# Entering the last stage of a three-stage kernel in another order: first tiles turned into two banks, two mixing tiles moved, VectorE's list rewritten

## What is computed

```python
x   = attention(q, k, v)              # 2 batches, 8 heads, window of 96 keys and 8 global keys
out = 0
for e in range(4):                    # the experts
    h = maximum(x @ w1[e], 0)         # 512 -> 1024
    out += p[:, e:e+1] * (h @ w2[e])  # 1024 -> 512
x  = out
h  = x @ w_in                         # the last stage: 512 -> 1024
sm = exp(h - max(h)) / (sum(exp(h - max(h))) + 1e-9)
s  = h * sm                           # softmax times its own argument ("solu")
ln = (s - mean(s)) / sqrt(var(s) + 1e-6) * g_ln
result = ln @ w_out                   # 1024 -> 512
```

## Time and profile before

| what | value |
|---|---|
| median of three runs | 760.61 us |
| the profiled execution, own time | 760.59 us |
| its span, first to last instruction | 758.8 us |
| TensorE busy | 745.1 us (98% of the span) |
| VectorE busy | 525.1 us (69%) |
| ScalarE busy | 220.9 us (29%) |
| GpSimd busy | 343.9 us (45%) |
| mean granted TensorE clock | 1.000 |
| last stage (first `up` to last instruction) | 605 to 758.8 us |

### The profile page before, as it was taken

How to read it: one execution, slowest core, us unless ns; L and a number is a source line. 1 busy time by engine, 2 the same in 40 slices (tenths; PEclk the granted TensorE clock), 3 DMA queues, 4 the chain that set the end, 5 groups by cost and what they waited for, 6 DMA issues and landing times.

```text
span 758.8 us, 12666 instructions
## 1 busy us (share of the span) xinstructions
PE 745.1 (98%) x3994; PEld 653.1 (86%) x3994; DVE 525.1 (69%) x1038; ACT 220.9 (29%) x418; POOL 343.9 (45%) x330
## 2 busy tenths in 40 slices
PE   9999999999999999999999999999999987999997
PEld 8888899889889988998898998989989865888885
DVE  5677767676666766666666666676677778867772
ACT  4677641111111111112111111111115643433331
POOL 4367546154451544516445164352645973442300
DMA  8746300101101001010010100100023000000001
GB/s 249 205 141 166 104 31 1 55 29 29 56 0 55 28 28 55 0 55 28 28 55 5 50 28 28 55 0 0 0 111 111 0 1 15 15 28 29 29 14 43
DMA packets 39103, 37.12 MB, mean 49 GB/s; under 512 B 14496, under 2 KB 31904, under 8 KB 39072
## 3 DMA queue, kind: packets, MB, share of 16 engines
q1 hardware_dynamic: 37472, 34.64, 14.8%
q10 hardware_dynamic: 1600, 2.10, 0.8%
HBM read 33.59 MB, written 3.15 MB: 48 GB/s over the span
## 4 chain that ended last, share of the span: by engine, by line
PE 94%; DVE 4%; issue 1%; ACT 0%; POOL 0%; POOLq 0%; DVEq 0%
PE y_ps L783 35%; PE p_ps L766 31%; PE o_ps L824 5%; PE s_ps L797 3%; PE pT_ps L807 3%; PE out_ps L1019 2%; PE out_ps L1021 2%; PE out_ps L1020 2%; PE up_ps L994 2%; PE up_ps L995 2%; PE up_ps L996 2%; PE lnT_ps L1006 1%; DVE ex L1721 1%; PE o_ps L901 1%; PE xt_ps L835 1%
## 5 line engine op out<-in xcount | busy, mean ns | idle before, releaser
L783 PE MATMUL y_ps<-w2s,hs 128*128 128x512 f32 x1152 | 289.3, 395 | 0.4 <-issue 0.3
L766 PE MATMUL p_ps<-xs,ws 128*128 128x384 f32 x1344 | 254.9, 336 | 0.0
L783 PEld LDWEIGHTS y_ps<-w2s,hs 128*128 128x128 f32 x1152 | 214.6, 188 | 41.7 <-issue 0.8
L766 PEld LDWEIGHTS p_ps<-xs,ws 128*128 128x128 f32 x1344 | 237.6, 188 | 11.0
L1430 DVE SCALAR_TENSOR_TENSOR acc<-y_ps,pr,acc 128x512 f32<-128x512 f32 x180 | 134.3, 748 | 80.1 <-PE y_ps L783 79.3
L1081 ACT ACTIVATE hs<-hs_sum 128x384 fp32r<-128x384 f32 x128 | 67.3, 526 | 354.1 <-DVE hs_sum L1398 238.9
L1417 DVE SCALAR_TENSOR_TENSOR hs<-hs_sum,hs 128x384 fp32r<-128x384 f32 x128 | 95.0, 752 | 3.8 <-ACT hs L1081 1.8
L546 POOL TENSOR_TENSOR ws_sum<-raw_sum 128x256 f32<-128x256 f32 x16 | 11.8, 738 | 147.8 <-PE p_ps L766 146.0
L577 POOL CAST w2s<-raw_sum 128x1024 fp32r<-128x1024 f32 x16 | 16.9, 1055 | 86.3 <-PE y_ps L783 86.3
L1094 ACT ACTIVATE neg_s<-neg_s,row 128x256 f32<-128x256 f32 (+1 forms) x96 | 42.1, 482 | 26.5 <-DVE row L1449 26.4
L1449 DVE CUSTOM_DVE_ANT_0 neg_s<-s_ps,bias 128x256 f32<-128x256 f32 (+1 forms) x96 | 34.3, 399 | 20.8 <-PE s_ps L797 18.6
(11 more groups left out here) (140 smaller groups left out, 967.0 us busy)
## 6 DMA issues: line engine op xcount, KB each, us to landing
raw_sum<-in_w SPq DMA_DIRECT2D x28, 512.0 KB, 3.5
qk<-in_qkW SPq DMA_DIRECT2D x24, 256.0 KB, 3.7
qk<-in_qkW SPq DMA_DIRECT2D x24, 128.0 KB, 4.1
v_sb<-in_v SPq DMA_DIRECT2D x16, 192.0 KB, 3.1
out<-o_sb SPq DMA_DIRECT2D x12, 256.0 KB, 2.0
raw_sum<-in_w ACTq DMA_DIRECT2D x4, 512.0 KB, 7.9
raw_sum<-in_w_in SPq DMA_DIRECT2D x1, 2048.0 KB, 7.6
wout_lo_a_sum<-in_w_out SPq DMA_DIRECT2D x1, 1792.0 KB, 7.7
```

The costliest lines, as they stand in the source:

```text
L766: mm = nc.tensor.matmul(bank, ws[slot][:, w, part, kk, :], xs[:, 2 * bt + kk, x, part, :], start=(kk == 0 and w == 1 and x == 1), stop=(kk ...
L783: mm = nc.tensor.matmul(y_ps[t % Y_BANKS][:, :], hs[bt][:, h, b, tok], w2s[slot][:, w, f, :], start=(f == 0 and h == 1 and w == 1), stop=( ...
```

## The change

- TensorE's loop over steps ends a turn earlier; its last four steps stand behind it as straight code. In step 31 `turn_x(0)` and `turn_x(1)` come between product 4 and product 3, the second into bank `up_ps[0]`.
- Only mix(31, 0) to mix(31, 3) stay ahead of the last stage; mix(31, 4) and mix(31, 5) come in pair 1 between up(1, 3) and down(0), into the banks `out_ps[1]` and `xr_ps`, and their add_up moves along. turn_ln(0) stands behind up(1, 4).
- The low parts c = 4 to 7 of w_out are made by VectorE (`wout_lo_part`, scaling in the same instruction) instead of GpSimd; ScalarE scales these parts in `wout_hi_part` and loses four `scale_wout`.
- GpSimd: x2_sums(1) and x2_los(1) directly behind those of pair 0; x2_sums(2) behind spread(1).
- ScalarE: relu_hi(31, 1) behind the first two x2_raws; ln_hi_part(0) ahead of x2_his(2, 1).
- VectorE's list of the last stage is written out as `first_pair`, `second_pair`, `pair` and `norms`. The late tile's h gets three halves (`h2_late`) that the pairs use in turn; late_left(1) comes ahead of solu_part(1).
- At the end ln_lo_part(10) comes ahead of normal(11), and turn_ln(11) between the two halves of down(10).

```diff
         with ExitStack() as same:
             wout_hi_b = sb(same, "wout_hi_b", [P, FC // 2, DM], F32R)
+            h2_late = sb(same, "h2_late", [P, 3, HALF])
...
-        h2 = sb(tail, "h2", [P, 2, F])
+        h2_early = sb(tail, "h2_early", [P, 2, HALF])
+        ln_lo0 = sb(tail, "ln_lo0", [P, FC, P], F32R)
...
-            ln_hi = sb(same, "ln_hi", [P, 2, FC, P], F32R, side="right")
-            ln_lo = sb(same, "ln_lo", [P, 2, FC, P], F32R, side="right")
+            ln_hi1 = sb(same, "ln_hi1", [P, FC, P], F32R, side="right")
+            ln_lo1 = sb(same, "ln_lo1", [P, FC, P], F32R, side="right")
...
+        with ExitStack() as same:
+            ln_hi0 = sb(same, "ln_hi0", [P, FC, P], F32R, side="right")
+        ln_hi, ln_lo = [ln_hi0, ln_hi1], [ln_lo0, ln_lo1]
...
+        def h2_at(s):
+
+            return h2_late[:, s // 2 % 2:s // 2 % 2 + 2, :] if s % 2 else h2_early[:, :, :]
+
+        def h2_half(q, m, half):
+
+            if m == 0:
+                return h2_early[:, half]
+            return h2_late[:, 1 if half else 2 * (q % 2)]
...
+        def turned_at(s):
+
+            return up_ps[0][:, :] if s == 1 else xr_ps[:, :]
+
+        def mixed_at(s, t):
+
+            if isinstance(s, int) and s == LAST and t > 3:
+                return out_ps[1][:, :] if t == 4 else xr_ps[:, :]
+            return y_ps[t % Y_BANKS][:, :]
...
-            for c in range(4):
+            for c in range(FC // 2):
                 split_wout(c)
-            x2_sums(0)
-            x2_los(0)
-            split_wout(4)
-            x2_sums(1)
-            x2_los(1)
-            for c in range(5, FC):
-                split_wout(c)
-            spread(0)
-            x2_sums(2)
-            spread(1)
-            x2_los(2)
-            for q in range(1, DUOS):
+            for q in range(2):
+                x2_sums(q)
+                x2_los(q)
+            for q in range(DUOS):
...
-                at_least(pe, acc_written, TILES * s + t + 1 - Y_BANKS)
+                if isinstance(s, int) and s == LAST and t == 5:
+                    pe.wait_ge(x2_raw, 6)
+                else:
+                    at_least(pe, acc_written, TILES * s + t + 1 - Y_BANKS + (isinstance(s, int) and s == LAST and t == 4))
...
+                if s == TILES:
+                    pe.wait_ge(acc_written, TILES * STEPS)
+                else:
+                    pe.wait_ge(acc_written, TILES * (LAST - 1 + s // TILES) + s % TILES + 1)
+                if s == 1:
+                    pe.wait_ge(p_sum, SETS * LAST + 3)
+                else:
+                    at_least(pe, x2_raw, s)
...
                 product(s, 4, i, g)
+                if isinstance(a, int) and s == LAST:
+                    turn_x(0)
+                    turn_x(1)
                 product(s, 3, i, g)
                 mix(last, 5, last_slot, last_bt, last_g)
...
-            with pe.Fori(1, STEPS // 4) as a:
+            with pe.Fori(1, STEPS // 4 - 1) as a:
                 for i in range(4):
                     step(a, i)
-            for t in range(TILES):
-                if t < 2:
-                    turn_x(t)
+            for i in range(4):
+                step(STEPS // 4 - 1, i)
+            for t in range(4):
                 mix(LAST, t, 1, 1, GROUPS - 1)
...
                 if s == 0:
-                    pe.wait_ge(acc_written, TILES * STEPS)
+                    pe.wait_ge(acc_written, TILES * LAST + 3)
...
                         if s == 0:
-                            pe.wait_ge(wout_ready, FC)
+                            pe.wait_ge(wout_ready, FC // 2)
+                            pe.wait_ge(wout_split, FC // 2)
+                        if s == 1:
+                            pe.wait_ge(acc_written, TILES * LAST + 5)
...
                 up(q, 5)
+                up(q, 4)
                 if q == 1:
                     turn_ln(0)
-                up(q, 4)
                 up(q, 3)
                 if q == 1:
+                    mix(LAST, 4, 1, 1, GROUPS - 1)
+                    mix(LAST, 5, 1, 1, GROUPS - 1)
                     down(0, 0)
                     turn_ln(1)
                     down(0, 1)
@@ -1053,8 +1092,9 @@
             down(TT - 3, 0)
             turn_ln(TT - 2)
             down(TT - 3, 1)
+            down(TT - 2, 0)
             turn_ln(TT - 1)
-            down(TT - 2, 0, 1)
+            down(TT - 2, 1)
             down(TT - 1, 0, 1)
...
             def wout_hi_part(c):
-                act.wait_ge(wout_scaled, c + 1)
-                nc.scalar.activation(wout_hi(c), wout_raw(c), ACT.Copy).then_inc(wouthi_ready, 1)
+                if c < FC // 2:
+                    act.wait_ge(wout_scaled, c + 1)
+                    nc.scalar.activation(wout_hi(c), wout_raw(c), ACT.Copy).then_inc(wouthi_ready, 1)
+                else:
+                    nc.scalar.activation(wout_hi(c), wout_raw(c), ACT.Copy, scale=gain_sb[:, c:c + 1]
+                                         ).then_inc(wouthi_ready, 1)
...
             relu_hi(LAST, 2, 1)
-            relu_hi(LAST, 1, 1)
-            scale_wout(4)
-            scale_wout(5)
...
             act.wait_ge(p_done, SETS * STEPS)
             x2_raws(0)
-            scale_wout(6)
-            scale_wout(7)
             x2_raws(1)
+            relu_hi(LAST, 1, 1)
             x2_his(0, 0)
-            for c in range(4, FC):
+            for c in range(FC // 2, FC - 2):
                 wout_hi_part(c)
             x2_his(0, 1)
+            for c in range(FC - 2, FC):
+                wout_hi_part(c)
...
                     ln_hi_part(late - 2)
+                if q == 1:
+                    ln_hi_part(0)
                 if q < DUOS - 1:
                     x2_his(q + 1, 1)
-                if q == 1:
-                    ln_hi_part(0)
                 exp_h(early)
                 if q == 1:
...
+            def wout_lo_part(c):
+
+                if c == FC // 2:
+                    dve.wait_ge(gain_loaded, 16)
+                dve.wait_ge(wouthi_ready, c + 1)
+                nc.vector.scalar_tensor_tensor(wout_lo(c), wout_raw(c), gain_sb[:, c:c + 1], f32(wout_hi(c)),
+                                               ALU.mult, ALU.subtract).then_inc(wout_split, 1)
+
+            for t in range(4):
                 add_up(LAST, t, 1, E - 1)
...
-            for q in range(DUOS):
-                early, late = 2 * q, 2 * q + 1
-                if q == 1:
-                    solu_part(0)
-                    solu_part(1)
-                    moments(0)
+            def first_pair():
+                wout_lo_part(4)
+                wout_lo_part(5)
+                late_left(0)
+                wout_lo_part(6)
+                second_up(0)
+                wout_lo_part(7)
+                third_up(0)
+                early_right(0)
+                fourth_up(0)
+                early_left(0)
+                late_right(0)
+
+            def second_pair():
+                solu_part(0)
+                moments(0)
+                late_left(1)
+                solu_part(1)
+                second_up(1)
+                normal(0)
+                third_up(1)
+                moments(1)
+                early_right(1)
+                ln_lo_part(0)
+                normal(1)
+                fourth_up(1)
+                add_up(LAST, 4, 1, E - 1)
+                early_left(1)
+                add_up(LAST, 5, 1, E - 1)
+                late_right(1)
+                ln_lo_part(1)
+
+            def pair(q):
                 late_left(q)
-                if q == 1:
-                    normal(0)
-                if q > 1:
-                    ln_lo_part(early - 2)
+                ln_lo_part(2 * q - 2)
                 second_up(q)
-                if q == 1:
-                    moments(1)
                 third_up(q)
-                if q == 1:
-                    ln_lo_part(0)
-                    normal(1)
                 early_right(q)
                 fourth_up(q)
                 early_left(q)
                 late_right(q)
-                if q > 0:
-                    ln_lo_part(late - 2)
-                    solu_part(early)
-                    moments(early)
-                    solu_part(late)
-                    normal(early)
-                    moments(late)
-                    normal(late)
-            ln_lo_part(TT - 2)
+                ln_lo_part(2 * q - 1)
+
+            def norms(q, more=None):
+                solu_part(2 * q)
+                moments(2 * q)
+                solu_part(2 * q + 1)
+                normal(2 * q)
+                moments(2 * q + 1)
+                if more is not None:
+                    ln_lo_part(more)
+                normal(2 * q + 1)
+
+            first_pair()
+            second_pair()
+            norms(1)
+            for q in range(2, DUOS - 1):
+                pair(q)
+                norms(q)
+            pair(DUOS - 1)
+            norms(DUOS - 1, more=TT - 2)
             ln_lo_part(TT - 1)
```

(24 more changed lines are left out.)

16 lines of the change are left out of this document (9 added, 7 removed).

## The result

| | before | after |
|---|---|---|
| median | 760.42 us (4 runs) | 756.49 us (4 runs) |
| all runs | 760.22 to 760.82 us | 755.00, 756.43, 756.56, 757.76 us |
| mean granted TensorE clock of these runs | 1.000 in the profiled one | 1.000, 0.998, 0.998, 0.995 |
| profiled execution, own time and span | 760.59 and 758.8 us | 757.76 and 756.0 us |
| ratio of the times, 95% interval | | 0.9947 [0.9928, 0.9966] |

The forecast was 755.8 us, range 754.4 to 758.4. The kernel is 3.9 us faster, and the time is inside the range. The runs spread over 2.8 us where those of before spread over 0.6. In these four the time goes with the mean granted clock: 755.00 at 1.000, 756.43 and 756.56 at 0.998, 757.76 at 0.995. That last one is the profiled execution, the slowest of the four.

What follows compares the result with a forecast made beforehand. TensorE was taken as the bound up to the last stage, where it waits 9.1 us in all. An earlier down(1), −3.1, and the end, −1.7, took 760.59 to 755.8 us; range 754.4 to 758.4 for 8 in 10.

Steps and rivals of the forecast that it cites:

- Entry: Ahead of up(0,1): TensorE ready about 601.5, x2_los(0) not; up(0,1) at 605.5 after 4.0 us idle.
- The term for wout_lo(4): VectorE's new wout_lo(4) ahead of x2_los(0)'s first part: 0.45 us on the path, bounds 0 and 0.7.
- First pair: wout_lo(5) to (7) push x2_los(1) from 616.1 to 617.2; second turn of pair 1 at 620.4, 1.4 us idle ahead.
- the sum: Whole kernel: 760.59 − 3.1 − 1.7 = 755.8 us, with no drop of the clock.
- Second pair: VectorE's shorter solu and new order, with `largest` held by GpSimd: down(1) at 638.6 instead of 641.73, −3.1 us.
- rival 1: Second pair: largest(2) misses its opening, waits for x2_los(2)'s second part, 1.9 us later: 757.7; chance 0.20.
- The end: Last tiles: ln_lo(10) goes first, down(11) starts at 748.2 instead of 749.93: −1.7 us, bounds 1.4 and 1.75.
- The clock: Rival: clock falls in the idle time at 601.5; short drop 756.2 to 757.7, chance 0.10; long 765, 0.04.
- The rule that the prediction sets against that reading: TensorE drops to half clock after being idle; set against the 4.0 us idle at 601.5, not in the forecast.
- the rival's own price: Pair 0 at 1.2 GHz: TensorE loses half the low level's time, 1.1 us of it free; short drop 0.4 to 1.9.
- 1.1 us of that is free: First pair: 1.1 us of low-clock loss costs nothing, since late_right(0) stands behind largest(0) until 617.2.
- the forecast's own range: Whole kernel: 755.0 to 756.8 us, from bounds of wout_lo, x2_los(1), largest(0) and the end; chance 0.57.

Runs made afterwards that it cites:

- e4: The changed kernel with two of GpSimd's four splits of w_out, split_wout(2) and (3), moved behind x2_los(0): 753.77 us, 0.9911.
- f3: The changed kernel with GpSimd's split_wout(2) and (3) moved behind x2_los(1): 752.98 us, 0.9906.
- f1: The kernel before with only the early turn_x(0) and turn_x(1) and TensorE's shorter loop: 760.39 us, 1.0.
- e2: The changed kernel with 34 unread transposes ahead of up(0,1), so that TensorE does not stand still there: 754.96 us, 0.9931.
- f2: e3 with the low parts 4 to 7 of w_out made by GpSimd again and scaled by ScalarE: 755.81 us, 0.9946.
- e3: The changed kernel with mixing tiles (31,4) and (31,5) and their add_up back ahead of the last stage: 754.57 us, 0.9924.
- e1: The kernel before with only the change's end: ln_lo_part(10) ahead of normal(11), turn_ln(11) between the halves of down(10): 758.45 us, 0.9975.

## Why the prediction was right or wrong

- **Entry, right.** TensorE was ready at 601.8 (forecast 601.5), GpSimd was not, up(0,1) came at 605.44. The term for wout_lo(4), 0.45, came out at 0.35: the first part of x2_los(0) took 2.20 us where it took 1.85. e4 and f3, with two splits fewer in front, show that the splits are what up(0,1) waits for; f1 that the early turns alone move nothing.
- **First pair, one term somewhat too large.** "x2_los(1) ended at 616.1 ... 617.2, bounds 616.4 and 618.0": at full clock (e2, on the axis of before) it ended at 616.9. The new wout_lo on VectorE push it by 0.8, not 1.1. Behind it the second turn came at 619.9 instead of 620.4 and down(1) at 638.1 instead of 638.6, a gain of 3.6 where 3.1 was forecast. That is most of why the clean runs (755.00, and e2) are 0.8 us under the sum; another 0.2 to 0.3 is that the sum starts from an execution of 760.59, where the kernel before has medians of 760.29 to 760.35 beside the experiments.
- **Second pair, right in its mechanism.** The order, the short solu, the three long `largest` and the end at a GpSimd instruction came as worked out; rival 1 did not happen in after or e2. One price was put in the wrong place: of the 2.2 us that the two solu save, the move of the low parts brings 1.0 and the order of the list the rest (f2). And the text had it that the tiles fill waits of 1.8 and 1.1 us, and also that VectorE would be held all the same without them. e3 shows the second statement to be the one that counts.
- **The end, right.** From down(1) to the end of the span e2 takes 753.1 − 637.73 = 115.4 us, before 758.8 − 641.73 = 117.1: −1.7, as forecast.
- **The clock, the step that failed.** "Against it: the earlier trace rows stayed at 1.00. Chance 0.10 short." It fell in the profiled run, and two of the other three runs, at a mean of 0.998, took 1.4 and 1.6 us more than the one at 1.000 (a mean does not say where the clock fell). One trace's reading was taken for a property of an idle time of that length; e1 and f1 show the same 2.4 us with the clock at 0.59 and 0.60 behind them. The rule that the prediction sets against that reading was the better guide. The Trainium skill, "TensorE: Matmul & The Clock Gate", "What's actually happening", adds of the rise at a kernel's start that its moment varies between runs, because the monitor runs freely and is not reset when a kernel starts. It does not say this of a fall within a kernel; that the four runs of after differ, 755.00 to 757.76, would fit it, and no run shows the cause.
- **The price of the clock, too low as well.** The low level lasted from 605.44 to about 611.1, 5.7 us of work. By the rival's own price that is 5.7 / 2 − 1.1 = 1.75 us. TensorE lost 2.5 us in it (from up(0,1) to up(0,2) 5.71 us, in e2 3.21), and 2.4 of them arrived at down(1). So "1.1 us of that is free" was wrong: the loss goes through turn_x(3) and x2_sums(1), where GpSimd waits 3.41 us and not 0.87, into x2_los(1) and from it into everything behind.
- So 755.8 against 756.49 is luck in part, two errors that partly cancel: 0.8 us too slow for a clean run, 1.5 too fast for the clock at the median. The median even lies in the forecast's own range, 755.0 to 756.8, which has no fall of the clock in it.

## What to carry to other kernels

Work taken off the bounding engine ahead of a hand-over only opens an idle time, on TensorE at the risk of the clock, unless the next operand is ready; so look first at what stands ahead of that operand in its own engine's list, and move that (here two splits, worth 3.5 us in f3 against after: 2.0 against e2, and the 1.5 of the clock). One execution at full clock does not clear an idle time of several us: ask what a low clock would delay, for it costs next to nothing beside a string on another engine (e1, e3) and nearly all of its loss on a chain that goes through TensorE (after, f4).
